# Low parts of the first network's weights made by accumulating DMAs and ScalarE casts, in a float32 kernel of attention and two networks

## The reference

```python
# q, k, v: (4, 8, 576, 64)
a = softmax(q_d k_d^T / 8) v_d          # on means of 4 neighbouring positions, repeated 4 times
b = softmax(q k^T / 8 where |i-j| < 4) v   # local attention: 7 keys a query
x = (a + b) as (2304, 512)
xn = x / sqrt(mean(x * x) + 1e-6) * rms_g
y = (silu(xn @ w_gate) * (xn @ w_val)) @ w_out   # first network, width 1536
h = max(y @ w_in, 0)
out = (s * h * h + b2) @ w_out2                  # second network, width 2048
```

## Time and profile before

| | us |
|---|---|
| median of 3 runs | 1024.13 (1022.45 to 1024.55) |
| the profiled execution, its own time | 1027.28 |
| its span, first to last instruction | 1025.2 |
| PE busy / DVE / ACT / POOL | 964.9 / 532.1 / 332.3 / 415.3 |

### The profile page before, as it was taken

How to read it: one execution, slowest core, us unless ns; L and a number is a source line. 1 busy time by engine, 2 the same in 40 slices (tenths; PEclk the granted TensorE clock), 3 DMA queues, 4 the chain that set the end, 5 groups by cost and what they waited for, 6 DMA issues and landing times.

```text
span 1025.2 us, 13271 instructions
## 1 busy us (share of the span) xinstructions
PE 964.9 (94%) x5080; PEld 782.2 (76%) x5080; DVE 532.1 (52%) x798; ACT 332.3 (32%) x718; POOL 415.3 (41%) x215
## 2 busy tenths in 40 slices
PE   4398899898999999999999999999999999999997
PEld 3276689797777667777777898887888888888896
DVE  4568777875675675555552133343443343333343
ACT  2243565324322341343123244322322232222232
POOL 4788879894886577544630254100000000000000
PEclk9999999999999999999999999999999999999999
DMA  9986347240422132102103233101100200100010
GB/s 252 283 244 195 95 126 223 85 127 19 131 64 84 37 118 77 41 18 70 31 6 123 83 125 103 42 1 42 42 1 6 77 1 1 55 7 1 1 42 21
DMA packets 55290, 79.41 MB, mean 77 GB/s; under 512 B 9852, under 2 KB 38108, under 8 KB 53948
## 3 DMA queue, kind: packets, MB, share of 16 engines
q1 hardware_dynamic: 53212, 73.86, 24.1%
q10 hardware_dynamic: 2016, 4.72, 1.2%
HBM read 67.05 MB, written 11.50 MB: 77 GB/s over the span
## 4 chain that ended last, share of the span: by engine, by line
PE 78%; POOL 7%; DVE 6%; issue 3%; DMA 2%; ACT 2%; SPq 1%; ACTq 0%; POOLq 0%; DVEq 0%
PE bank L717 24%; PE bank L848 6%; PE bank L849 6%; PE bank L850 6%; PE bank L866 6%; PE bank L867 6%; PE bank L868 6%; PE bank L758 4%; PE bank L756 4%; PE bank L757 4%; POOL prod L520 3%; POOL prod L534 2%; DMA rawk<-in_k_dram 2%; PE bank L1481 1%; PE bank L1514 1%
## 5 line engine op out<-in xcount | busy, mean ns | idle before, releaser
L520 POOL TENSOR_TENSOR prod<-qs,ks 128x896 f32<-128x896 f32 x80 | 180.5, 2279 | 77.0 <-DVE sc L540 63.7
L534 POOL TENSOR_TENSOR prod<-sc,vs 128x896 f32<-128x896 f32 x80 | 149.6, 1987 | 56.4 <-DVE x L550 36.8
L887 DVE SCALAR_TENSOR_TENSOR r<-bank,r 128x512 f32<-128x512 f32 (+1 forms) x80 | 51.1, 638 | 183.7 <-ACT r L875 183.7
L850 PE MATMUL bank<-y_h,w2i_l 128*128 128x512 f32 (+1 forms) x320 | 117.7, 368 | 0.0
L717 PE MATMUL bank<-x_h,wv_h 128*128 128x256 f32 (+1 forms) x288 | 104.4, 378 | 8.4 <-DVE h_l L784 7.5
L756 PE MATMUL bank<-h_h,wo_h 128*128 128x256 f32 (+1 forms) x288 | 107.0, 371 | 0.4 <-issue 0.4
L778 DVE TENSOR_TENSOR bank<-bank,u 128x256 f32<-128x256 f32 (+1 forms) x72 | 40.5, 562 | 125.4 <-PE bank L717 119.0
L875 ACT ACTIVATE r<-bank 128x512 f32<-128x512 f32 (+1 forms) x80 | 44.4, 556 | 183.7 <-PE bank L850 183.0
L540 DVE TENSOR_REDUCE sc<-prod 128x14 f32<-128x896 f32 x80 | 85.4, 1078 | 31.4 <-POOL prod L520 31.4
L758 PE MATMUL bank<-h_h,wo_l 128*128 128x256 f32 (+1 forms) x288 | 97.5, 338 | 0.0
L757 PE MATMUL bank<-h_l,wo_h 128*128 128x256 f32 (+1 forms) x288 | 96.8, 336 | 0.0
(11 more groups left out here) (132 smaller groups left out, 1959.0 us busy)
## 6 DMA issues: line engine op xcount, KB each, us to landing
raww<-in_moe_w_out_dram SPq DMA_DIRECT2D x14, 512.0 KB, 3.7
ks<-in_k_dram SPq DMA_DIRECT2D x16, 280.0 KB
vs<-in_v_dram SPq DMA_DIRECT2D x16, 280.0 KB, 4.7
raww<-in_moe_w_in_dram SPq DMA_DIRECT2D x8, 512.0 KB, 3.7
y_raw<-y_scr SPq DMA_DIRECT2D x4, 1024.0 KB, 4.8
out_dram<-o_st SPq DMA_DIRECT2D x16, 256.0 KB, 2.8
rawq<-in_q_dram SPq DMA_DIRECT2D x3, 1152.0 KB, 13.4
rawk<-in_k_dram SPq DMA_DIRECT2D x3, 1152.0 KB, 14.3
```

The lines of the kernel that those rows point to most:

```text
L520: pool.tensor_tensor(dst, qv, kv, ALU.mult).then_inc(prod_ready, 1)
L534: pool.tensor_tensor(dst, pv, vv, ALU.mult).then_inc(prod_ready, 1)
L850: last = pe.matmul(o, w2i_l[:, m, kk, :], y_h[t % 2][:, kk, 0:w], start=False, stop=kk == DT - 1)
```

## The change

All 18 weight pieces of the first network lose their subtraction. `weight_hi` writes the high part negated (scale -1). A DMA issued from GpSimd (`weight_rest`) adds it onto the raw piece in place, which leaves the rest in `raww`. ScalarE then casts that rest, negated, to the low part (`weight_low`), and frees the slot. Gate and value thus come out negated: `silu` gets scale -1, and the product with the negated `w_out` is positive again. The gate and value weights are stored with each piece contiguous. Tile 1's reductions, softmax, `add_pooled` and first `squares` stand some steps earlier in VectorE's and ScalarE's lists. SyncE issues the q and k loads of tile 2's first two heads between the last pieces, ahead of them rather than behind.

```diff
-LO_AT = {0: (4,), 1: (6,), 2: (8,), 3: (10,), 5: (12,), 6: (14,), 7: (16,), 8: (17,)}
-QK1_AT = {1: (6, 7), 2: (8,), 3: (9,), 4: (10, 11), 5: (12,), 6: (13,), 7: (14,), 8: (15,)}
+LOW_AT = {0: (4, 5), 1: (6, 7), 2: (8,), 3: (9, 10), 4: (11,), 5: (12, 13), 6: (14,), 7: (15, 16), 8: (17,)}
+REST_AT = {("qk", 0): (3,), ("qk", 6): (4, 5), ("qk", 9): (6, 7), ("qk", 11): (8,), ("qk", 13): (9, 10), ("qk", 15): (11, 12, 13, 14),
+           ("pv", 0): (15,), ("pv", 1): (16,), ("pv", 3): (17,)}
+QK1_AT = {0: (7, 8), 1: (9, 10), 2: (11, 12), 3: (13, 14), 4: (15,)}
...
-PV1_AT = {(0, 10): (0,), (0, 11): (1, 2), (1, 0): (3, 4), (1, 1): (5, 6, 7), (1, 2): (8, 9), (1, 3): (10, 11, 12), (1, 4): (13, 14, 15)}
+PV1_AT = {(0, 7): (0, 1), (0, 8): (2, 3), (0, 9): (4, 5), (0, 10): (6, 7), (0, 11): (8, 9), (1, 0): (10, 11), (1, 1): (12, 13), (1, 2): (14, 15)}
...
-            act.activation(hi, staged(n, rows), ACT.Copy).then_inc(w_hi, 1)
+            act.activation(hi, staged(n, rows), ACT.Copy, scale=-1.0 if n < NW1 else 1.0).then_inc(w_hi, 1)
+
+        def weight_rest(pool, n):
...
+            pool.wait_ge(w_hi, n + 1)
+            pool.dma_start(staged(n, rows), f32(hi), accum_op=ALU.add).then_inc(w_rest[n % SLOTS], 16)
+
+        def weight_low(act, n):
...
+            act.wait_ge(w_rest[n % SLOTS], 16 * (n // SLOTS + 1))
...
+            act.activation(lo, staged(n, rows), ACT.Copy, scale=-1.0).then_inc(w_lo[n % SLOTS], 1)
...
+                if n in (10, 11, 13):
+                    weight_rest(pool, (10, 11, 13).index(n))
...
+                if n == 24:
+                    weight_low(act, 0)
                 if n == 25:
                     weight_hi(act, 3)
+                    weight_low(act, 1)
+                if n == 26:
+                    weight_low(act, 2)
+                if n == 29:
+                    weight_low(act, 3)
...
-                if n == 30:
+                if n == 29:
                     qk_reduce(dve, 1, 0)
                     qk_reduce(dve, 1, 1)
+                if n == 30:
+                    qk_reduce(dve, 1, 2)
+                    qk_reduce(dve, 1, 3)
                 if n == 31:
-                    qk_reduce(dve, 1, 2)
-            qk_reduce(dve, 1, 3)
-            weight_lo(dve, 3)
+                    qk_reduce(dve, 1, 4)
+            qk_reduce(dve, 1, 5)
             dve.wait_ge(small_loaded, 48)
             split_lo(dve, 0, 0)
             split_lo(dve, 0, 1)
-            qk_reduce(dve, 1, 4)
-            qk_reduce(dve, 1, 5)
+            qk_reduce(dve, 1, 6)
...
-                    if m == 8:
+                    if m == 5:
                         softmax_max(dve, 1)
-                    if m == 9:
+                    if m == 6:
                         softmax_norm(dve, 1)
```

More of the change, by code:

```diff
@@ L169, in build @@
         gv_start = at[0]
-        wg_h = place(at, "wg_h", [P, M1, DT, P], F32R)
-        wv_h = place(at, "wv_h", [P, M1, DT, P], F32R)
+        wg_h = place(at, "wg_h", [P, M1 // 2, DT, 2, P], F32R)
+        wv_h = place(at, "wv_h", [P, M1 // 2, DT, 2, P], F32R)
         gl_start = at[0]
-        wg_l = place(at, "wg_l", [P, M1, DT, P], BF16)
-        wv_l = place(at, "wv_l", [P, M1, DT, P], BF16)
+        wg_l = place(at, "wg_l", [P, M1 // 2, DT, 2, P], BF16)
+        wv_l = place(at, "wv_l", [P, M1 // 2, DT, 2, P], BF16)
         att_start = at[0]
@@ L304, in build @@
         w_hi, w_lo = sem("w_hi"), [sem(f"w_lo{i}") for i in range(SLOTS)]
+        w_rest = [sem(f"w_rest{i}") for i in range(SLOTS)]
         xt_ps, xh_done, xl_done, xb_done = sem("xt_ps"), sem("xh_done"), sem("xl_done"), sem("xb_done")
@@ L335, in piece @@
                 w, hi, lo = (w_gate, wg_h, wg_l) if kind == "gate" else (w_val, wv_h, wv_l)
-                return (w.rearrange("(k p) f -> p k f", p=P)[:, :, m * P:(m + 2) * P], two(hi, m), two(lo, m), DT)
+                return (w.rearrange("(k p) f -> p k f", p=P)[:, :, m * P:(m + 2) * P], hi[:, j, :, :, :], lo[:, j, :, :, :], DT)
             kind, j = second_order[n - NW1]
@@ L390, in weight_hi @@
                 room_hi(act, n)
-            act.activation(hi, staged(n, rows), ACT.Copy).then_inc(w_hi, 1)
+            act.activation(hi, staged(n, rows), ACT.Copy, scale=-1.0 if n < NW1 else 1.0).then_inc(w_hi, 1)
+        def weight_rest(pool, n):
+            src, hi, lo, rows = piece(n)
+            pool.wait_ge(w_hi, n + 1)
+            pool.dma_start(staged(n, rows), f32(hi), accum_op=ALU.add).then_inc(w_rest[n % SLOTS], 16)
+        def weight_low(act, n):
+            src, hi, lo, rows = piece(n)
+            act.wait_ge(w_rest[n % SLOTS], 16 * (n // SLOTS + 1))
+            if n == FIRST_ORDER.index(("val", M1 // 4)):
+                act.wait_ge(prod_ready, pv_at(0, 15) + 1)
+            act.activation(lo, staged(n, rows), ACT.Copy, scale=-1.0).then_inc(w_lo[n % SLOTS], 1)
         def weight_lo(eng, n):
@@ L396, in weight_lo @@
             eng.wait_ge(w_hi, n + 1)
[L397 to L400, removed]
+            room_lo(eng, n)
             eng.tensor_tensor(lo, staged(n, rows), f32(hi), ALU.subtract).then_inc(w_lo[n % SLOTS], 1)
@@ L716, in first_in @@
                     pe.wait_ge(xb_done, ROUND0[c + 1])
-                last = pe.matmul(o[:, 0:w], wt[:, m, kk, :], xs[:, kk, cols], start=i == 0, stop=i == 3 * DT - 1)
+                last = pe.matmul(o[:, 0:w], wt[:, m // 2, kk, m % 2, :], xs[:, kk, cols], start=i == 0, stop=i == 3 * DT - 1)
             return last
@@ L765, in silu @@
             wait(act, hf_ready, s - 1 if w < W_ and m else s)
-            act.activation(u[:, u_part(s)], gate_bank(s)[:, 0:w], ACT.Silu).then_inc(u_ready, 1)
+            act.activation(u[:, u_part(s)], gate_bank(s)[:, 0:w], ACT.Silu, scale=-1.0).then_inc(u_ready, 1)
         def hidden_hi(act, s):
@@ L1026, in _ @@
             load_piece(sp, 13)
+            load_qk(sp, 1, 7)
             load_piece(sp, 14)
-            load_qk(sp, 1, 7)
+            load_qk(sp, 2, 0)
             load_piece(sp, 15)
+            load_qk(sp, 2, 1)
             load_piece(sp, 16)
@@ L1037, in _ @@
                     load_v(sp, a, 1)
-                if a + 1 < TILES:
+                if 1 < a < TILES - 1:
                     load_qk(sp, a + 1, 0)
@@ L1108, in _ @@
                 pv_mult(pool, 0, n)
-            weight_lo(pool, 0)
-            weight_lo(pool, 1)
-            weight_lo(pool, 2)
+                if n in (10, 11, 13):
+                    weight_rest(pool, (10, 11, 13).index(n))
             for n in range(16):
[L1113 to L1122, removed]
                 qk_mult(pool, 1, n)
-            weight_lo(pool, 15)
+                for i in REST_AT.get(("qk", n), ()):
+                    weight_rest(pool, i)
             for a in range(1, TILES):
@@ L1133, in _ @@
                     pv_mult(pool, a, n)
+                    if a == 1:
+                        for i in REST_AT.get(("pv", n), ()):
+                            weight_rest(pool, i)
             for n in range(NW1, NW1 + NW2):
@@ L1199, in _ @@
                 late = 1 if c == 2 else 0
-                if c == 0 and m == 9:
+                if c == 0 and m == 6:
                     softmax_exp(act, 1)
-                if c == 1 and m == 3:
+                if c == 1 and m == 2:
                     squares(act, 1, 0)
@@ L1235, in _ @@
                         weight_hi(act, n)
+                    for n in LOW_AT.get(m, ()):
+                        weight_low(act, n)
                 if c == 1 and m == 6:
@@ L1396, in _ @@
                         split_lo(dve, 1, m - 1)
-                    for n in LO_AT.get(m, ()):
-                        weight_lo(dve, n)
                     for n in QK1_AT.get(m, ()):
                         qk_reduce(dve, 1, n)
-                    if m == 8:
+                    if m == 5:
                         softmax_max(dve, 1)
-                    if m == 9:
+                    if m == 6:
                         softmax_norm(dve, 1)
@@ L1409, in _ @@
                 if c == 1:
-                    if m == 2:
+                    if m == 1:
                         add_pooled(dve, 1, 0)
-                    if m == 4:
+                    if m == 3:
                         add_pooled(dve, 1, 1)
```

## The result

| | median of 4 runs | lowest to highest | first 512-wide matmul |
|---|---|---|---|
| before | 1023.29 us | 1022.43 to 1024.55 | 263.22 |
| after | 1050.21 us | 1047.22 to 1052.41 | 287.70 |

The ratio is 1.026 (95%: 1.0231 to 1.0289), 26.9 us slower. The sign was forecast, the size was not: 7.6 us were expected, and the time lies outside the range. The profiled execution took 1049.86 us (span 1048.1). That is 22.6 us above the profiled execution of before, which was itself 4 us above its median.

The account below looks back on a forecast made before the run. TensorE was taken as the bound. A 512-wide part 5.3 us later, 1.7 of clock and 0.6 at `val`(16) made +7.6 us: 1034.9 against the profiled execution, 1031.7 for the median, range 1020.6 to 1042.

Parts of the forecast that it names:

- The bound and the stretch: TensorE bounds the kernel; only time until the first 512-wide matmul at 263.22 can move, with 58.2 us behind gate 11.
- Issue on GpSimd: Each of eighteen DMA issues on GpSimd takes 1.0 us, between bounds of 0.40 and 2.4.
- rival 3: Issue as dear as a subtraction (2.4 us) or transfer twice a load: much slower, 1044 to 1050, chance 0.15.
- Casts 1.0: Each of eighteen added low-part casts on ScalarE takes 1.0 us.
- the vanished wait at 240: TensorE's 4.44 us wait ending at 240.00 goes, with 1.7 us of clock given back.
- The start: x_l's matmuls, at 147.35 before, start 2.5 us later because six reductions stand ahead of chunk 0's `split_lo`.
- The walk up to `silu`(2): Stepping through the engines' lists in the first 256-wide chunk, `silu`(1) ends at 159.2 and `silu`(2) at 166.7.
- The transfer: Each adding transfer within SBUF takes 4.6 us from issue to landing, 3.6 behind the issue; bounds 2.2 and 9.2.
- SyncE's queue: SyncE's two moved loads for tile 2 are cheap, needed only at the end of tile 1's qk products; nothing charged.
- The clock: 1.7 us of lost TensorE clock charged for a new 5.6 us wait before gate 10, and 1.7 given back.
- The sum: Gate 11 14.5 us late, 2.5 start and 12.0 new waits less old; altogether +5.3 + 1.7 + 0.6 = +7.6 us.
- Rival 1: Transfers are cheap (2.2 us in all) and ScalarE keeps up: faster, down to 1020.6 us, chance 0.22.

Follow-up runs that it names:

- e4: The changed kernel with plain copies in place of the adding DMAs, so the addition is left out: 1040.5 us, ratio 1.016 to before.
- e5: The changed kernel with plain copies and SyncE's q and k loads moved ahead of the weight pieces: 1031.8 us, ratio 1.008 to before.
- e8: The kernel before with adding DMAs for five late pieces only and tile 1's attention one step earlier: 1032.1 us, ratio 1.007 to before.
- e10: The kernel before with the earlier attention order (alone 1046.0 us) and SyncE's q and k loads ahead of pieces, subtractions kept: 1055.0 us.
- e9: The kernel before with only tile 1's k and q loads of heads 5 to 7 ahead of pieces 8, 10 and 12: 1036.0 us.
- e12: The changed kernel with adding DMAs over only the first half of each partition's row: 1041.9 us, ratio 1.017 to before.

## Why the prediction was right or wrong

- **The bound and the stretch: right.** All of the loss lies ahead of the first 512-wide matmul. Behind gate 11, now at 230.00, come 287.70 - 230.00 = 57.7 us; 58.2 were taken, and no wait of 4.4 us is left behind 220.
- **Issue on GpSimd, 1.0 us taken: right.** It took 0.85 to 1.46 us. The starving of descriptor generation that the Trainium skill warns of (SBUF — State Buffer, summary of rules) is stated there for VectorE's 2x and 4x modes, a condition that rival 3 left out. No issue here came near the 2.4 us of rival 3; what makes some longer than 0.85 was not taken apart.
- **Casts 1.0, the vanished wait at 240: right.**
- **The start, 2.5 us taken: too large.** x_l's matmuls begin at 145.07 against 147.35. This execution's lead was 3.4 us in GpSimd's first pv product (82.67 against 86.10) and 2.1 in TensorE's third transposes (12.01 against 14.12), so the start moved by 1.1 us at most.
- **The walk up to `silu`(2): right in the number by luck.** From the end of `silu`(1) to that of `silu`(2) it took 12.0 us and not 7.5, behind a transfer of 10.68 us; the early start hid it.
- **The transfer, 4.6 us taken: mis-sized, the larger part.** Medians of 6.4 to 7.8 us, up to 10.7. "No slack for the queues" and the remark that the engines' share "nears 1" (it became 0.80, and 0.94 in single windows) were right and not carried into the sum. The upper bound of 9.2 us, from reading two tiles, was the nearer end; rival 3's transfer half (1050) gives the measured time, but by luck: it had the whole loss come from landings of 9.2 us, and SyncE's list made a part of it. Copies, which in e4 land in 3.9 to 4.5 us, are 9.8 us faster, and with no transfer at all it is 23.9.
- **SyncE's queue, charged nothing: the step that failed.** "SyncE's two loads for tile 2 are cheap" looked at the two moved loads, and not at the loads of heads 5, 6 and 7, which stand in SyncE's list behind pieces that now wait for low casts. GpSimd waited 24.6 us for k; at least 7.7 of them are the list's, and 10.9 the slow landing on full DMA engines, which the sum had at nothing too. Tile 1's softmax ended at 211.4 and not near 194. The better list is worth 6.8 us, with copies 8.6.
- **Together.** e5, with copies and the better list, takes 1031.8 us, forecast 1031.7. From there the record goes up by 8.6 for the list and 9.8 for the adding transfer to 1050.2; these are differences of the same runs, so that they close proves nothing. That the first number fits to 0.1 us is luck: the landings in e5 have a median of 5.5 us over loads and transfers and 7.7 us of waits for k are left, against 4.6 and nothing in the walk. The two terms also act on each other: taken with the adding transfer, the list is worth 6.8.
- **The clock: too small.** 1.7 us were charged for one long wait, and as many taken as given back, so the sum had nothing for it. The granted clock from 146 to 196 us was 0.81, and a matmul of 128x256 took 0.41 us in parts of that stretch, against 0.28. The same 861 matmuls kept TensorE busy for 114.87 us instead of 107.04, which makes this 7.8 us. It comes behind the waits, as at 167.45; no run here varied it by itself.
- **The sum: a slip of 0.8 us.** The waits listed before the gates up to 11 add up to 14.2 us; less the 1.4 that stood there before (0.8 for a low part, 0.4 for an issue, 0.2 for `hidden_lo`) that is 12.8, where the text has 12.0.
- **Rival 1, transfers that are cheap enough: half right.** Even with none at all the kernel takes 1026.3; only with the list mended too does it reach 1017.6.

For the DMA's own time the estimate from the fit in the Trainium skill (DMA: Bandwidth & Descriptors, anatomy of a GpSimd-issued DMA) is 3.2 us for 512 KB. Plain copies in e4 landed 2.9 us from their issue at the fastest and 4.0 in the median; the fastest one is near the estimate. For one that adds, the medians are 6.4 to 7.8 us, twice the estimate and more.

What stays open is how the loss of the adding transfers splits between their own length and what they take from the loads beside them. One without neighbours (piece 8, issued at 171.39, with the DMA share at 1.03 from 173 to 175 us) landed in 4.5 us, so 1.9 to 3.3 us of the medians is company. e8's five still had medians of 6.0 to 6.4.

## What to carry to other kernels

Follow each in-order list once for every wait that the change puts into it, and ask what stands behind: here it was not the new DMA's own queue but the loads behind a slot that it frees late. Price a transfer by the engines' time that it takes from those already running, and where the sum of shares nears 1, reckon with late landings for all of them, the small loads too: k's took 10.9 us here. The best place of a load in such a list is no property of the list: the same list gained 7 to 9 us where transfers made the low parts and cost 9 where subtractions did (e10), and one like it cost 11 to 12 in the kernel before (e9). Price a row of long waits with the clock that follows them: 18.9 us more of waiting came with 7.8 us of slower matmuls.

## What the runs showed of the hardware

- A DMA within SBUF that adds to its target took 2.85 us of all 16 engines for 512 KB, 1.9 times the 1.5 us of a plain copy (e4). Half the bytes (e12) took 1.56.
- Issue to landing of such an adding DMA was 4.5 us for one without neighbours and 10.7 at most.
- One issue on GpSimd of an adding DMA for a tile of 128 x 4 KB took 0.85 to 1.46 us, that of a plain copy of the same tile (e4) 0.53 to 0.73.
- The granted clock of TensorE was 0.50 in a window of 10 us in which it was busy for 5.0, and 0.83 in one with 4.4 busy; it was 1.00 from 230 us, behind the last of the waits for `silu`, to the first 512-wide matmul at 287.70.
